# The last GEMM of an attention-MoE-MoE chain on one core: seven-product blocks over both halves of K in units 2 and 3

## What is computed

```python
def _attn_ref(q, k, v, cap):            # batch 2, 12 heads, seq 448, head_dim 64
    scores = cap * np.tanh(scale * np.matmul(q, k.transpose(0, 1, 3, 2)) / cap)
    ...softmax over the last axis...
    return np.matmul(attn, v)
def _moe_ref(x, w_in, w_out):           # x 896 x 768, w_in 768 x 2048, w_out 2048 x 768
    h = x @ w_in
    return np.maximum(0.01 * h, h) @ w_out
def _moe2_ref(x, w_gate, w_val, w_out, rms_g):   # w_gate, w_val 768 x 1536, w_out 1536 x 768
    xn = x / np.sqrt(np.mean(x * x, axis=-1, keepdims=True) + 1e-06) * rms_g
    g, val = xn @ w_gate, xn @ w_val
    return (g / (1.0 + np.exp(-g)) * val) @ w_out
```

## Time and profile before

| | us |
|---|---|
| median of three executions | 571.8 (571.29 to 572.05) |
| the profiled execution, its own time | 573.29 |
| its span, first to last instruction | 571.5 |
| TensorE busy | 565.1 (99%) |
| VectorE busy | 390.2 (68%) |
| GpSimd busy | 310.5 (54%) |
| ScalarE busy | 287.1 (50%) |
| granted TensorE clock, mean of the span | 0.999 |

### The profile page before, as it was taken

How to read it: one execution, slowest core, us unless ns; L and a number is a source line. 1 busy time by engine, 2 the same in 40 slices (tenths; PEclk the granted TensorE clock), 3 DMA queues, 4 the chain that set the end, 5 groups by cost and what they waited for, 6 DMA issues and landing times.

```text
span 571.5 us, 7775 instructions
## 1 busy us (share of the span) xinstructions
PE 565.1 (99%) x2724; PEld 475.1 (83%) x2724; DVE 390.2 (68%) x543; ACT 287.1 (50%) x495; POOL 310.5 (54%) x269
## 2 busy tenths in 40 slices
PE   9999999999999999999999999999999999999997
PEld 5544554688999999999999989999999999989996
DVE  4479897695555454335975599988888989991513
ACT  6889888226444564345644456444444453631210
POOL 1035463569566553335652577777868785554440
PEclk9999999999999999999999999999999999999999
DMA  6355432213111141110210011122111111041401
GB/s 170 96 173 164 107 111 62 51 44 111 57 55 56 60 135 55 57 56 28 84 55 29 1 56 57 56 83 84 57 55 56 56 55 57 0 143 42 148 18 64
DMA packets 29717, 41.48 MB, mean 73 GB/s; under 512 B 17008, under 2 KB 18672, under 8 KB 29680
## 3 DMA queue, kind: packets, MB, share of 16 engines
q1 hardware_dynamic: 29536, 40.99, 23.2%
q10 hardware_dynamic: 144, 0.00, 0.0%
HBM read 38.15 MB, written 2.80 MB: 72 GB/s over the span
## 4 chain that ended last, share of the span: by engine, by line
PE 96%; DVE 2%; issue 1%; ACT 1%; ACTq 0%; DVEq 0%
PE ps L1509 51%; PE ps L1576 21%; PE ps L1432 9%; PE ps L1686 7%; PE ps L1420 4%; PE ps L1438 2%; PE ps L1424 1%; PE ps L1518 1%; DVE act_full L1263 1%; ACT x_hi L835 0%; DVE x_raw L911 0%; DVE x_lo L1267 0%; PE ps L1628 0%; DVE sums_eps L917 0%; PE ps L1651 0%
## 5 line engine op out<-in xcount | busy, mean ns | idle before, releaser
L538 POOL TENSOR_TENSOR w_lo<-w_raw,w_hi 128x384 fp32r<-128x384 f32 x113 | 132.8, 1180 | 157.7 <-ACT w_hi L648 157.2
L1509 PE MATMUL ps<-x_hi,w_hi 128*128 128x448 f32 x474 | 174.5, 368 | 0.0
L1509 PE MATMUL ps<-x_hi,w_lo 128*128 128x448 f32 x474 | 173.6, 366 | 0.0
L1509 PE MATMUL ps<-x_lo,w_hi 128*128 128x448 f32 x474 | 173.6, 366 | 0.0
L538 POOL TENSOR_TENSOR w_lo<-s_sum,w_hi 128x384 fp32r<-128x384 f32 x92 | 104.8, 1150 | 55.5 <-ACT w_hi L648 55.5
L1509 PEld LDWEIGHTS ps<-x_hi,w_hi 128*128 128x128 f32 x474 | 89.0, 188 | 9.3 <-issue 1.3
L1509 PEld LDWEIGHTS ps<-x_hi,w_lo 128*128 128x128 f32 x474 | 89.0, 188 | 7.8
L1509 PEld LDWEIGHTS ps<-x_lo,w_hi 128*128 128x128 f32 x474 | 89.0, 188 | 7.7
L648 ACT ACTIVATE w_hi<-s_sum 128x384 fp32r<-128x384 f32 x92 | 47.8, 523 | 91.5 <-PE ps L1509 69.5
L648 ACT ACTIVATE w_hi<-w_raw 128x384 fp32r<-128x384 f32 x113 | 57.7, 515 | 32.9 <-PE ps L1686 18.5
L1432 PE MATMUL ps<-probs,v_ones 128*65 128x448 f32 x144 | 56.6, 541 | 0.2 <-DVE x_raw L911 0.2
(11 more groups left out here) (162 smaller groups left out, 938.5 us busy)
## 6 DMA issues: line engine op xcount, KB each, us to landing
w_raw<-in_w_out SPq DMA_DIRECT2D x28, 384.0 KB, 3.3
w_raw<-in_w_in SPq DMA_DIRECT2D x16, 384.0 KB, 4.1
qk_raw<-in_qk SPq DMA_DIRECT2D x11, 480.0 KB, 4.2
w_raw<-in_w_gate SPq DMA_DIRECT2D x12, 384.0 KB, 3.1
w_raw<-in_w_val SPq DMA_DIRECT2D x12, 384.0 KB, 3.7
v_ones<-in_v SPq DMA_DIRECT2D x12, 224.0 KB, 3.3
recip_row<-recips SPq DMA_DIRECT2D x12, 224.0 KB, 3.5
out<-sq SPq DMA_DIRECT2D x6, 224.0 KB, 1.9
```

The lines of the kernel that those rows point to most:

```text
L538: pool.tensor_tensor(w_lo[:, c], source, w_hi[:, c].bitcast(F32), ALU.subtract).then_inc(w_lo_done, 1)
L1509: last = pe.matmul(ps[:, base(s) + to, 0:S], w[:, w_c], x, start=(j in (P1, P5, P7, P6) and c == 0 and first), stop=(c == KH - 1 and w is ...
```

## The change

In units 2 and 3 of the last GEMM both halves of K go by the seven products: a product then has a part 0 (early half of K) and a part 1 (late half), which add into the same bank, 14 x 9 matmuls a unit. In unit 1 the halves change roles: the early half (part 0) goes by the seven products, the late half (part 1) plainly. VectorE's sums `T1` to `T4` are needed for both parts; those of part 0 are made in the value units (`EARLY_SUMS`), those of part 1 in unit 1. `w_raw` is loaded with part 0 first. The number of weight slices goes from 33 to 39, and `s_part` gets a part. Part 0's B11, T1 and T3 are split early (ScalarE `early_upper`, GpSimd `early_lower`), all else by `z_hi` and `z_lo`. The core of the diff:

```diff
-    LAST_ORDER = [P1, P5, PA, PB, P7, PC, P6, PD, P3, P2, P4]
-    F0 = N2 // 2
+    LAST_ITEMS = [[(P1, 0), (P5, 0), (P7, 0), (P6, 0), (PA, 1), (PC, 1), (P3, 0), (P2, 0), (P4, 0), (PB, 1), (PD, 1)],
+                  [(j, part) for j in (P1, P5, P7, P6, P3, P2, P4) for part in (0, 1)],
+                  [(j, part) for j in (P1, P5, P7, P6, P3, P4, P2) for part in (0, 1)]]
...
+        EARLY_SPLITS = {U1 + 4: (0,), U1 + 5: (1,), U1 + 6: (2,), U1 + 8: (3, 4), U1 + 9: (5, 6), U1 + 10: (7, 8)}
+
+        EARLY_SUMS = {U1 + 2: [(T1, 0)], U1 + 3: [(T1, 1)], U1 + 4: [(T1, 2)], U1 + 5: [(T3, 0)], U1 + 6: [(T3, 1), (T2, 0)],
+                      U1 + 7: [(T3, 2), (T2, 1)], U1 + 8: [(T2, 2), (T4, 0)], U1 + 9: [(T4, 1)], U1 + 10: [(T4, 2)]}
+
+        Z = [(part, blk, c) for part, blk in ((1, B11), (1, B12), (0, T2), (0, B22), (0, B21), (0, T4), (1, B21), (1, B22),
+                                              (1, T1), (1, T3), (1, T2), (1, T4)) for c in range(KH)]
...
-                for k, (row, half) in enumerate(((m, 1), (m + KH, 1), (m, 0), (m + KH, 0))):
-                    load_raw(r + k, w_out2[row, half])
+                for k, (row, part) in enumerate(((m, 0), (m + KH, 0), (m, 1), (m + KH, 1))):
+                    load_raw(r + k, w_out2[row, part])
```

ScalarE's queue from the last value unit on:

```diff
+            last_weights(s, (P1, 0))
+            z_upper(1, B11)
+            last_weights(s, (P5, 0))
+            z_upper(1, B12)
+            last_weights(s, (P7, 0))
+            z_upper(0, T2)
+            last_weights(s, (P6, 0))
             silu(s - 1, 1)
+            last_weights(s, (PA, 1))
+            z_upper(0, B22)
+            silu(s - 1, 0)
+            last_weights(s, (PC, 1))
+            z_upper(0, B21)
+            last_weights(s, (P3, 0))
             keep_p1(s)
+            last_weights(s, (P2, 0))
+            z_upper(0, T4)
+            last_weights(s, (P4, 0))
+            z_upper(1, B21)
+            z_upper(1, B22)
+            last_weights(s, (PB, 1), (PD, 1))
+            s = UNITS + 1
+            last_weights(s, (P1, 0), (P1, 1))
+            z_upper(1, T1)
+            last_weights(s, (P5, 0))
+            z_upper(1, T3)
+            last_weights(s, (P5, 1), (P7, 0))
+            z_upper(1, T2)
+            last_weights(s, (P7, 1), (P6, 0), (P6, 1))
+            z_upper(1, T4)
+            keep_p1(s)
+            last_weights(s, *LAST_ITEMS[1][8:])
```

A weight sum waits for the slice that it overwrites, and VectorE's queue (what stands in it from the last value unit to unit 2; lines that both kernels have are kept as context):

```diff
+            def s_part(s, j, part=0):
+
+                r, made = raw_of(s) + 2 * part, sums_before(s, part)
+                if part == 1:
+                    dve.wait_ge(w_lo_done, widx(s, j) + 1)
+                elif s > 0:
+                    dve.wait_ge(w_lo_done, widx(s - 1, j, last_part(s - 1)) + 1)
...
             s = UNITS - 1
             s_part(s + 1, P5)
             s_part(s + 1, P7)
             take_p5(s)
+            s_part(s + 1, P6)
+            s_part(s + 1, P3)
             take_p7(s)
+            z_lower(1, B11)
             take_p6(s)
             value_22(s)
+            z_lo(1, B12, 0)
             gate_sum(s)
             gate_12(s)
+            z_lo(1, B12, 1)
+            z_lo(1, B12, 2)
+            gate_11(s)
             weighted_1(s)
+            z_lower(0, T2)
             value_21(s)
             weighted_0(s)
 
             s = UNITS
+            z_lo(0, B22, 0)
+            z_lo(0, B22, 1)
+            take_p5(s)
+            z_lo(0, B22, 2)
             take_p7(s)
+            z_lo(0, B21, 0)
+            z_lo(0, B21, 1)
             take_p6(s)
+            z_lo(0, B21, 2)
+            z_lower(0, T4)
+            z_lower(1, B21)
+            z_lower(1, B22)
+            z_sums(T1)
+            s_parts(s + 1)
+            z_lower(1, T1)
+            z_sums(T3)
+            z_sums(T2)
+            s_part(s + 1, P5, 1)
+            result_11(s)
+            result_12(s)
+            z_lower(1, T3)
+            result_21(s)
+            result_22(s)
+            z_sums(T4)
+            s = UNITS + 1
+            s_part(s, P7, 1)
+            z_lower(1, T2)
+            s_part(s, P6, 1)
+            s_part(s, P3, 1)
+            take_p5(s)
+            z_lower(1, T4)
+            take_p7(s)
+            take_p6(s)
             result_22(s)
             s_parts(s + 1)
             result_12(s)
```

`z_lower`, `z_sums` and `s_parts` are three, three and four operations. The outputs of a unit are stored in the order of `RESULTS`; `result_11` needs one operation (bank A holds its whole sum) where it needed two, and the last unit ends with it. TensorE:

```diff
+            def last_product(s, j, part):
+                n = widx(s, j, part)
+                pe.wait_ge(w_lo_done, n + 1)
+                if part == 0:
+                    bank_free(s, j)
+                for c in range(KH):
+                    if (s, part) == (UNITS, 0) and j in (B11, T1, T3):
+                        pe.wait_ge(early_lo_done, early_count[j, c])
+                    elif (s, part) in ((UNITS, 0), (UNITS + 1, 1)):
+                        pe.wait_ge(z_lo_done, z_count[part, j, c])
...
+            for j in (P1, P5, P7, P6):
+                last_product(UNITS, j, 0)
+            plain_half(0)
+            for j in (P3, P2, P4):
+                last_product(UNITS, j, 0)
+            plain_half(1)
+            for s in range(UNITS + 1, LAST):
+                for j, part in LAST_ITEMS[s - UNITS]:
+                    last_product(s, j, part)
```

More of the change, by code:

```diff
@@ L376, in plain_lo @@
[L376 to L391, removed]
+        B_TILE = {B11: (0, 0), B12: (0, 1), T3: (0, 1), B21: (KH, 0), B22: (KH, 1)}
@@ new lines, in z_lower, with z_sums, wait_result, result_11 @@
+            def z_lower(part, blk):
+                for c in range(KH):
+                    z_lo(part, blk, c)
+            def z_sums(blk):
+                for c in range(KH):
+                    z_sum(1, blk, c)
+            def wait_result(s, j, piece):
+                if s == UNITS:
+                    dve.wait_ge(prod_done, count[widx(s, piece, 1)])
+                else:
+                    dve.wait_ge(prod_done, count[widx(s, j, 1)])
+            def result_11(s):
+                dve.wait_ge(act_done, 2 * N2)
+                at_least(dve, out_sem[O11], 16 * (s - UNITS))
+                wait_result(s, P2, PB)
+                dve.tensor_tensor(sq[0][:, :], bank(s, BANK_A), r_bc[:, cols(0)], ALU.mult).then_inc(o11_done, 1)
@@ L1287, in result_11 @@
[L1287 to L1298 removed]
+                dve.tensor_tensor(a_t[s % 2][:, :], a_t[s % 2][:, :], r_bc[:, cols(1)], ALU.mult).then_inc(o22_done, 1)
@@ L1387, in _ @@
             result_12(s)
+            s_part(s + 1, P5, 1)
+            s_part(s + 1, P7, 1)
             result_11(s)
             result_21(s)
-            for s in range(UNITS + 1, LAST):
-                take_p5(s)
-                take_p7(s)
-                take_p6(s)
-                result_22(s)
-                if s + 1 < LAST:
-                    s_parts(s + 1)
-                result_12(s)
-                result_11(s)
-                result_21(s)
+            s = UNITS + 2
+            s_part(s, P6, 1)
+            s_part(s, P3, 1)
+            take_p5(s)
+            take_p7(s)
+            take_p6(s)
+            result_22(s)
+            result_12(s)
+            result_21(s)
+            result_11(s)
         @block.tensor
@@ L1504, in product @@
                     w_c = slice(n % 7 * HALF + c * 128, n % 7 * HALF + (c + 1) * 128)
[L1505 to L1510 removed]
+                    for w, x in ((w_hi, x_hi), (w_hi, x_lo), (w_lo, x_hi)):
+                        last = pe.matmul(ps[:, base(s) + BANK_OF[j], 0:S], w[:, w_c], x[:, xs(j, c)],
+                                         start=(j in (P1, P5, P7, P6) and c == 0 and w is w_hi and x is x_hi),
                                          stop=(c == KH - 1 and w is w_lo), skip_group_check=(j in (P3, P2, P4)))
```

441 lines of the change are left out of this document (195 added, 246 removed).

## The result

| | before | after |
|---|---|---|
| median, same chip, six executions each | 571.92 | 575.59 |
| lowest and highest | 570.73 to 573.36 | 574.06 to 576.26 |
| profiled execution: its time, its span | 573.29, 571.5 | 575.06, 573.3 |
| granted TensorE clock, mean of the span | 0.999 | 0.993 |

The ratio is 1.0061 with an interval of [1.0042, 1.0080]: 3.5 slower (2.4 to 4.6), where the forecast was 0.6. 575.59 lies 0.1 above the range as written; counted from this chip's before (571.92 for the 571.8 of the forecast) it is 575.5, the range's upper end.

A forecast was written before the change was run, and what follows sets the result against it. TensorE, busy 99%, bounds the kernel; its savings of 3.7 + 1.6 + 0.66 go on about 6.5 of waiting for VectorE. Last matmul 1.3 later, tail 0.66 shorter: 0.6 later, 572.4 for 571.8, range 567.0 to 575.5.

The forecast's parts named there:

- t0: Start on VectorE of the weight sum for P7 part 1 in unit 2, forecast at 522.4; sets the time while over 516.
- the walk: VectorE's queue counted from 473.16: 38.9 of its own operations plus 10.3 of collisions with GpSimd, ending at 522.4.
- likeliest case: The forecast of 572.4 from counting through VectorE's queue, own range 570.6 to 574.0, chance 0.52.
- every collision full: Rival: all 16 GpSimd subtractions cost VectorE 0.80 each, time 574.9; chance 0.21, slower.
- start of the walked queue: Where before issues z_t1 on VectorE and the change has a T4 sum: 473.16, as in before.
- t0 to the start of P3 part 0: Unit 2: weight split lets TensorE go on 2.5 after t0; with a later wait for take_p5, 9.7 in all.
- P3 to the end of the last matmul: Units 2 and 3: 180 matmuls at 0.2042 plus 0.17, with no wait longer than their spacing.
- own-time: What VectorE's 63 tile operations and 9 weight sums need without collisions: 33.7 + 4.2 + 1.0 = 38.9.
- GpSimd is passed over: Rival: runs of ready two-input VectorE operations keep GpSimd out, six collisions (4.8) vanish, time 567.6; chance 0.20.
- the early sums cost nothing: Value units: one or two extra VectorE sums each, costed at nothing; the first 2.2 of take_p5's lateness free.
- the wait of 1.6 before P3: Unit 2: TensorE stands 1.6 more before P3 part 0, waiting for take_p5 in VectorE's queue.
- hidden with about 1 to spare: Unit 3's weight loads go out about 6 before TensorE wants them and land 3.3 after issue; 2 later costs 1.

The follow-up runs named there:

- late_results: The changed kernel with unit 1's results moved in VectorE's queue behind weight sums and the sums T4: 572.76, 1.0015 of before.
- short_split: The changed kernel with GpSimd making low parts of only 64 of 384 columns of the last GEMM's weights: 566.45, 0.9887 of before.
- early_p5: The changed kernel with take_p5 of unit 1 moved ahead of two low parts in VectorE's queue: 574.41, 1.0041 of before.
- before_stall3: The kernel before with take_p6 of unit 1 moved behind three low parts of B21, lengthening its one stall: 574.46, 1.0042 of before.

## Why the prediction was right, and where it was short

The mechanism was right: VectorE's queue has no room, t0 comes within 1.1 of the walk (523.5 for 522.4), and what TensorE saves is waited away. late_results and short_split show it by moving t0. The size was not: 3.5 and not 0.6. The likeliest case's own range ended at 574.0, and it gave "same" over "slower" 0.34 to 0.16. The wide range reached 575.5 only by the rival "every collision full" (574.9). Its number is nearest, but its mechanism is not what happened, so that the range reached just far enough is luck. The likeliest case said the last matmul ends at 569.0; by before's clock it ends at 571.5 (570.14 + 1.40). By the prediction's own steps:

| step | predicted | measured (before's clock) | late by |
|---|---|---|---|
| start of the walked queue | 473.16 | 473.90 | 0.7 |
| its length, to t0 | 49.2 | 49.6 | 0.4 |
| t0 to the start of P3 part 0 | 9.7 | 10.1 | 0.4 |
| P3 to the end of the last matmul | 36.9 | 38.0 | 1.1 |

That is 2.6. The end behind the last matmul is shorter by 0.55 for 0.66, so the whole is 0.6 + 2.6 + 0.1 = 3.3, which is what the two traces give; the ratio gives 3.5.

**The walked queue.** The windows of VectorE and of GpSimd alone, from its start to t0:

```profile
472.50:522.06 49.56, 49.18 (x73) 0.97 0.21 67
...
472.50:522.06 49.56, 18.70 (x16) 0.97 0.21 67
```

Sixteen subtractions, 49.18 of 49.56 busy: the count held, and over the own-time of 38.9 they cost 0.67 each, for 0.65. (How the 49.6 divides into own-time and collisions is known only as short_split gives it.) The rival "GpSimd is passed over" (44.4 for this queue) fails as a rule, and so does "every collision full" (51.7).

**The start.** I wrote that the early sums cost nothing, and if they did, 2.2 of lateness was free for `take_p5`. That looked at TensorE, which indeed never waits before 490. But the end is set by VectorE's queue, and there every delay counts from the moment when it has no gap left. Its timeline where the last value unit begins, and GpSimd's beside it:

```profile
469.33 0.62 DVE L1271 TENSOR_TENSOR u<-ps,u 128x448 f32<-128x448 f32 x1 [0.19 <-PE ps L1580]
469.87 1.34 DVE L1277 TENSOR_TENSOR act_full<-a_t,sq 128x448 f32<-128x448 f32 x1
471.13 1.44 DVE L1283 TENSOR_TENSOR act_full<-u,sq 128x448 f32<-128x448 f32 x1
472.50 1.44 DVE L1313 TENSOR_TENSOR sq_acc<-act_full 128x448 f32<-128x448 f32 x1
```
```profile
469.71 3.74 POOL L575 TENSOR_TENSOR w_lo<-w_raw,w_hi 128x384 fp32r<-128x384 f32 x3
```

The same place before:

```profile
471.27 0.61 DVE L1230 TENSOR_TENSOR act_full<-a_t,sq 128x448 f32<-128x448 f32 x1
```
```profile
470.28 2.48 POOL L538 TENSOR_TENSOR w_lo<-w_raw,w_hi 128x384 fp32r<-128x384 f32 x2 [1.58 <-ACT w_hi L648]
```

The operation at 469.33 is on time (470.73 before). Before, the first subtraction started 0.99 ahead of the first `weighted` operation and was nearly done; now it starts 0.16 ahead, with one of the early splits of the change right in front of it (468.09 to 469.63), and two more follow. The `weighted` operation takes 1.34 where it took 0.61. That is the 0.7: not the sums themselves, but GpSimd at another moment. It was not tried by a run.

**t0 to P3.** TensorE goes on 3.06 behind t0, not 2.5. The rows of the weight's low part and of VectorE beside it:

```profile
L575 POOL TENSOR_TENSOR w_lo<-s_sum,w_hi x1: 1760/1760/1760, 523.3 to 523.3; 128x384 fp32r<-128x384 f32 x1
```
```profile
522.53 1.69 DVE L1322 TENSOR_TENSOR act_lo<-act_full,x_hi 128x448 fp32r<-128x448 f32 x3
```

I had put it behind one low part of `T2`. It came inside three that were all ready, at full stride (1.69 for three), and got through only after the last: 1.76 instead of 1.02, as in the earlier trace rows. So the passed-over case does exist, once, and at the place for which TensorE waits. (The Trainium skill, "SBUF — State Buffer", section "SBUF: two separate sides": whoever starts first holds the shared ports for its whole instruction. The trace agrees, but says more: the waiting one need not come next.) The clock had fallen, and 27 matmuls took 7.0 instead of 5.5, which covers the wait of 1.6 before P3: `take_p5` ended at 531.70, 9.6 behind t0 as walked, and TensorE was there at 532.16. At P3 the late start and the second tail thus cost 0.4, and at the end nothing: the chain shown above reaches 545.94 without a matmul, so a TensorE that came 0.4 earlier to P3 would have stood 0.4 longer in unit 3. The 1.5 of the table's last two rows belong to what follows. The first tail ends in the second stall and costs nothing, as early_p5 shows.

**P3 to the end.** The step that failed most: the loads of unit 3, which I had as hidden with about 1 to spare. The third of them, for P1 part 1, goes out when GpSimd is done with its buffer at 538.20, 6.8 before TensorE wants it (545.03). I gave it the 3.3 of the earlier trace rows, a median over all loads of the program. Here four of 384 KB leave within 2.15, and this one landed after 5.56; then ScalarE 0.53 and GpSimd 1.46 (a collision, 1.02 alone). 6.8 - 5.6 - 0.6 - 1.5 = -0.9. The trace of before had a nearer number, that of its own four loads for unit 3, issued within 1.86. Landing times of the four, before and then after:

```profile
DMA to landing us min/median/max: 3.0/4.6/5.3
```
```profile
DMA to landing us min/median/max: 3.3/5.0/6.1
```

The forecast had named the price of such a miss (2 later costs 1); its chance was not in the sum.

**What was not in the text at all** is the clock. I took each stall to cost its idle time, which is so for the one of the earlier trace rows (1.30 idle, clock 1.00 behind it). The two long stalls of after each have a tail of 1.5 to 1.6, and the waits behind them absorb both. before_stall3, where nothing waits later, pays for its tail in full. (One sum of the prediction is off by 0.1: 180 matmuls from 483.25 end at 520.0, not 519.9. Nothing rests on it.)

**What stays open.** What decides whether the clock falls with an idle stretch of 1.8 to 2.3 was not settled. What the load costs (0.9 of standing, up to 1.5 with the 0.4 above) and what the moved subtraction costs (0.7) is read from the traces; no version was tried that sends the loads of unit 3 earlier or moves the early splits.

## What to carry to other kernels

When an engine's queue sets the end, every edit in front of it counts, also one that "only" uses up its last gap or lets another engine collide with it once more: ask of each step whether the binding queue is late, not whether TensorE is. Take the landing time of a load from loads issued in the same company, not from the median of the program. And treat a TensorE stall of two microseconds as one that may cost three and a half: before counting on its removal, look whether a later wait would absorb it, and put the work that releases TensorE ahead of the work that only finishes a result; here that order alone turned 3.5 slower into 2.8 faster.

## What the runs showed of the hardware

- TensorE idle for 0.69, 0.76, 1.00 and 1.30 went on at full speed in these profiles; with 1.94, 1.95, 2.27, 2.56, 2.81 and 4.88 the granted clock went to its lower level. It fell 0.5 to 1.4 after TensorE had gone on (1.94, 1.95, 2.27, 2.81), 0.3 before that (2.56) and 2.2 before that (4.88), and stayed low for 3.4, with 4.88 for 6.8. With 1.85 it did not fall in the profiled execution, and the mean clocks say that in five or six of the others it did.
- A fall costs some 1.4 to 1.6 by the times of executions of one kernel, 1.5 to 1.6 by the spacing of its matmuls, and 2.2 by spacing with the idle time of 4.88.
- GpSimd subtractions of 384 columns beside VectorE's work cost VectorE 8.3 over a queue of 72 operations, against ones of 64 columns.
- A GpSimd subtraction asked for during three back-to-back ready VectorE operations can wait for all three (1.76 for 1.02).
- A 384 KB load lands 3.3 after its issue by the median of the program before, and 4.6 (before) and 5.0 (after) by the median of the four for unit 3, issued within 1.86 and 2.15.
